# Four small reorderings where the attention of a fused attention, convolution-gate and channel-mix kernel hands over to its projections

## What is computed

```python
# 1. attention, 16 heads in all, masked by a hash bucket of q and k (6 bits)
mask = q_bucket[:, :, :, None] == k_bucket[:, :, None, :]
scores = np.where(mask, scale * np.matmul(q, k.transpose(0, 1, 3, 2)), -1e9)
attn = softmax(scores);  x = merge_heads(attn @ v)
# 2. gated projection: causal convolution over 5 tokens gives the gate
gate = sigmoid(sum_k conv_w[k] * x[t - 4 + k])
x = (gate * (x @ w_val)) @ w_out
# 3. channel mix with the previous token
xk = mu_k * x + (1 - mu_k) * x_prev;  xr = mu_r * x + (1 - mu_r) * x_prev
k = relu(xk @ w_k);  r = sigmoid(xr @ w_r)
out = r * ((k * k) @ w_v)
```

## Time and profile before

| | |
|---|---|
| runs of the kernel (3) | 488.40, 488.49, 489.15 us; median 488.49 |
| profiled execution | 488.57 us, its span 486.8 us |
| TensorE busy | 475.1 us, 98% of the span |
| VectorE, ScalarE, GpSimd busy | 350.5, 279.2, 257.9 us |
| granted TensorE clock | 1.00 in all stretches |

### The profile page before, as it was taken

How to read it: one execution, slowest core, us unless ns; L and a number is a source line. 1 busy time by engine, 2 the same in 40 slices (tenths; PEclk the granted TensorE clock), 3 DMA queues, 4 the chain that set the end, 5 groups by cost and what they waited for, 6 DMA issues and landing times.

```text
span 486.8 us, 9484 instructions
## 1 busy us (share of the span) xinstructions
PE 475.1 (98%) x3541; PEld 403.4 (83%) x3541; DVE 350.5 (72%) x611; ACT 279.2 (57%) x597; POOL 257.9 (53%) x254
## 2 busy tenths in 40 slices
PE   8899999999999999999999999999999999999997
PEld 6766677676676676667679998999999999999997
DVE  4887897988889888887687986884786588226211
ACT  4977878887787887876645533451442353244230
POOL 5795547284463746451267546464456458246140
PEclk9999999999999999999999999999999999999999
DMA  6210310304031030200220001001000000000101
GB/s 229 66 55 18 116 37 25 114 16 136 16 97 58 1 135 18 72 18 18 88 86 1 3 1 43 1 1 45 2 2 32 12 2 19 27 1 12 34 1 43
DMA packets 10557, 20.69 MB, mean 42 GB/s; under 512 B 1680, under 2 KB 6928, under 8 KB 10512
## 3 DMA queue, kind: packets, MB, share of 16 engines
q1 hardware_dynamic: 10224, 19.94, 12.5%
q10 hardware_dynamic: 288, 0.15, 0.1%
HBM read 16.94 MB, written 3.15 MB: 41 GB/s over the span
## 4 chain that ended last, share of the span: by engine, by line
PE 78%; DVE 11%; issue 4%; ACT 3%; DMA 2%; POOL 1%; SPq 0%; DVEq 0%; ACTq 0%; POOLq 0%
PE ps L717 28%; PE ps L705 14%; PE ps L725 12%; PE ps L681 10%; PE ps L670 10%; DVE gate L898 2%; DMA raw_k<-kT 2%; ACT probs L482 2%; PE ps L691 2%; DVE tmp_a L971 1%; DVE negmax L855 1%; DVE pt L862 1%; DVE tmp_b L969 1%; PE ps L653 1%; DVE x L888 1%
## 5 line engine op out<-in xcount | busy, mean ns | idle before, releaser
L855 DVE TENSOR_REDUCE negmax<-ps 128x1 f32<-128x768 f32 x96 | 91.7, 956 | 23.7 <-PE ps L670 22.6
L670 PE MATMUL ps<-k,q 128*128 128x384 f32 x384 | 91.9, 361 | 3.1 <-ACT probs L482 2.5
L482 ACT ACTIVATE probs<-ps,negmax 128x768 f32<-128x768 f32 x96 | 86.6, 902 | 9.8 <-DVE negmax L855 9.4
L681 PE MATMUL ps<-ident,probs 128*128 128x128 f32 x576 | 82.4, 275 | 1.9 <-ACT pt L490 0.7
L681 PEld LDWEIGHTS ps<-ident,probs 128*128 128x128 f32 x576 | 66.7, 140 | 12.8 <-DVE pt L862 4.7
L670 PEld LDWEIGHTS ps<-k,q 128*128 128x128 f32 x384 | 62.7, 189 | 14.8 <-ACT probs L482 10.2
L705 PE MATMUL ps<-pt,vals 128*64 128x384 f32 x384 | 68.8, 494 | 0.0
L436 POOL TENSOR_TENSOR h_lo<-tmp_b,h_hi 128x256 fp32r<-128x256 f32 x48 | 38.7, 812 | 45.9 <-ACT h_hi L584 45.9
L490 ACT ACTIVATE pt<-ps 128x384 f32<-128x384 f32 x96 | 47.0, 489 | 19.7 <-PE ps L681 15.9
L862 DVE COPY pt<-ps 128x384 f32<-128x384 f32 x96 | 52.2, 543 | 3.7 <-PE ps L681 3.7
L725 PE MATMUL ps<-h_hi,w_hi 128*128 128x256 f32 x192 | 54.3, 283 | 0.0
(11 more groups left out here) (87 smaller groups left out, 1124.8 us busy)
## 6 DMA issues: line engine op xcount, KB each, us to landing
w_raw<-w SPq DMA_DIRECT2D x8, 640.0 KB, 6.9
raw_q<-qT SPq DMA_DIRECT2D x8, 384.0 KB, 5.8
raw_k<-kT SPq DMA_DIRECT2D x8, 384.0 KB, 3.5
vals<-v SPq DMA_DIRECT2D x16, 192.0 KB, 2.3
out<-w_raw SPq DMA_DIRECT2D x24, 128.0 KB, 1.7
w_raw<-w SPq DMA_DIRECT2D x4, 512.0 KB, 3.2
codes_b<-codes ACTq DMA_DIRECT2D x1, 128.0 KB, 4.1
proj_bd<-proj ACTq DMA_DIRECT2D x1, 16.0 KB, 3.3
```

Of the source, the lines that this page charges most:

```text
L482: act.activation(probs[par][:, :], score[par], ACT.Exp, bias=negmax[:, t:t + 1], accum_out=sums[:, t, 0:1]).then_inc(exp_done, 1)
L670: last = pe.matmul(ps[:, 2 * par + half, 0:HALF], qq[h][:, q], kk[h][:, half * HALF:(half + 1) * HALF], start=first, stop=not first)
L681: last = pe.transpose(tbank[u][:, k * P:(k + 1) * P], probs[g % 2][:, kt * P:(kt + 1) * P], ident[:, :])
L855: dve.tensor_reduce(negmax[:, t:t + 1], score[g % 2], AX.XY, ALU.max, negate=True).then_inc(max_done, 1)
```

## The change

1. *Gate tile ahead of transposes (TensorE).* The first value tile of chunk 0 goes from behind the transposes of step 94 to behind those of step 93, so ahead of those of step 94. It gets a wait for the exponential of step 94, whose score banks it overwrites.
2. *Low parts on GpSimd.* The four low parts of y of chunk 0 go from VectorE to GpSimd, two ahead of each of its two pieces of w_v's low part.
3. *Keys do not wait for the receptance (TensorE).* `s_k` waits for seven of the eight low parts of the mixtures, `s_r` for all eight.
4. *Tanh behind the next second stage (ScalarE), left taps between outputs (VectorE).* `tanh_gate(c + 2)` goes behind `s_out(c + 1)`. The left taps (12 in chunk 0, 4 in chunks 1 to 3) go from the end of `s_k` into `s_v`: a quarter ahead of each output product.

```diff
@@ block.gpsimd
+            y_low(0, 0)
+            y_low(0, 1)
             w2_low(0)
+            y_low(0, 2)
+            y_low(0, 3)
             w2_low(1)
             pool.wait_ge(mm["val"], DT)
             x_low(1)
@@ block.scalar
+                if c + 1 < CHUNKS:
+                    s_out(c + 1)
                 if c + 2 < CHUNKS:
                     tanh_gate(c + 2)
-                if c + 1 < CHUNKS:
-                    s_out(c + 1)
@@ block.tensor
-                if i == LAST and t >= TILES - 2:
+                if i == LAST and t >= TILES - 3:
                     pe.wait_ge(xlo_done, 1)
-                    s_val_tile(0, 2 * (t % 2))
-                    s_val_tile(0, 2 * (t % 2) + 1)
+                    if t < TILES - 1:
+                        pe.wait_ge(exp_done, NHEADS * KT - 1)
+                        s_val_tile(0, t - (TILES - 3))
+                    else:
+                        s_val_tile(0, 2)
+                        s_val_tile(0, 3)
@@ s_k, s_r
-                pe.wait_ge(mixlo_done, (c + 1) * 2 * DT)
+                pe.wait_ge(mixlo_done, (c + 1) * 2 * DT - 1)
...
             def s_r(c):
+                pe.wait_ge(mixlo_done, (c + 1) * 2 * DT)
@@ block.vector
+            def tap_rate(c):
+                return 2 if c else 1
...
-                if c + 2 < CHUNKS:
-                    for n in range(taps * FT, DT * TAPS):
-                        convolve_tap(c + 2, n // TAPS, n % TAPS)
 
             def s_v(c):
-                dve.wait_ge(rec_done, c + 1)
+                left = DT * TAPS - tap_rate(c) * FT
                 for m in range(DT):
+                    if c + 2 < CHUNKS:
+                        for n in range(DT * TAPS - left + left * m // DT, DT * TAPS - left + left * (m + 1) // DT):
+                            convolve_tap(c + 2, n // TAPS, n % TAPS)
+                    if m == 0:
+                        dve.wait_ge(rec_done, c + 1)
                     dve.wait_ge(mm["v"], c * DT + m + 1)
...
             gated(0, 1)
             normalise(NHEADS - 2)
-            y_low(0)
-            y_low(1)
             gated(0, 2)
             gated(0, 3)
-            y_low(2)
-            y_low(3)
             normalise(NHEADS - 1)
```

More of the change, by code:

```diff
@@ L418, in gates, with y_low @@
                     .then_inc(gate_done, 1)
+            def y_low(c, m):
+                pool.wait_ge(yhi_done, c * DT + m + 1)
+                pool.tensor_tensor(y_lo[:, m, :], tmp_a[:, m % 2, :], y_hi[:, m, :], ALU.subtract)\
+                    .then_inc(ylo_done, 1)
             def s_val(c):
                 for m in range(DT):
-                    pool.wait_ge(yhi_done, c * DT + m + 1)
-                    pool.tensor_tensor(y_lo[:, m, :], tmp_a[:, m % 2, :], y_hi[:, m, :], ALU.subtract)\
-                        .then_inc(ylo_done, 1)
+                    y_low(c, m)
             def s_out(c):
@@ L955, in s_val @@
                     gated(c, m)
[L957 to L960, removed]
             def s_out(c):
@@ L982, in save_last @@
                     dve.memset(z[:, :, 0:1], 0.0).then_inc(hist_done, 1)
+            def tap_rate(c):
+                return 2 if c else 1
             def s_k(c):
-                taps = 2 if c else 1
+                taps = tap_rate(c)
                 for m in range(FT):
```

## The result

The changed kernel takes 485.91 us (median of 6 runs, 485.69 to 486.08) against 488.50 of the kernel before (6 runs): a ratio of 0.9944, 95% interval 0.9934 to 0.9954, 2.6 us or 0.5% faster.

The account below looks back on a forecast made before the run. TensorE was taken as the bound, with 2.5 us of waits to remove. Terms: -1.15 at the keys, -1.2 at chunk 2's value tiles, +0.6 new wait, sum -1.75 us, giving 486.8 us; range 486.0 to 487.9.

Parts of the forecast that it names:

- What bounds the kernel, and where the gains lie: TensorE bounds, busy 146.88 of 146.92 us from 337.25 us on; its three earlier waits, together 2.5 us, are the most to gain.
- Gate tile: TensorE, step 94's transposes: a value tile of 1.4 us fills the 0.67 us wait for a copy; gain 0.7 us.
- Low parts on GpSimd: Chunk 0's y low parts cost 0.74 us each on GpSimd, ready 1.6 us early; on VectorE all but 0.15 us is lost.
- The mixing chain moves 0.4 us, not 0.7: VectorE's first difference of chunk 0, held by GpSimd's x low part, ends at 252.9 instead of 253.26; keys start at 261.0.
- Tanh and taps, the gain: TensorE, first gate-value tile of chunk 2: output products come in time, so the 1.20 us wait goes; gain 1.2 us.
- New wait: 0.6 us: TensorE, output projection of chunk 2 near 317.6: waits for ScalarE's receptance tanh because the gate comes late; bounds 0 and 1.1.
- GpSimd in its own way: Rival, chance 0.07: y low parts on GpSimd take 1.21 us each, keys start 0.75 us later than before; 488.7 us.
- Taps held up: Rival, chance 0.05: the 12 taps between VectorE's outputs take 0.98 us each, new wait 6.2 us; 492.4 us.
- The gate eating the second gain: Rival, chance 0.14: the new wait at chunk 2's output projection is 1.1 us or more, start gives only 0.74; 487.7 us.

Follow-up runs that it names:

- the delayed gates: Changed kernel with two or five extra unused multiplications ahead of the last tap of chunk 0's output stage on VectorE: 486.50 us with two, 487.15 us with five.
- the two kernels with a wait near 2 us: The changed kernel without the tanh and taps moved (488.22 us), and the kernel before with only keys not waiting for the last receptance low part (490.37 us).

## Why the prediction was wrong

By its steps:

- **What bounds the kernel, and where the gains lie: right.** All three waits that it read the earlier trace rows are gone, the view of TensorE's waits has none beyond 340 us, and the gain changes there by less than 0.1 us (2.78 to 2.71).
- **Gate tile: right in kind, too small.** 0.87 us instead of 0.7. The term was the 0.67 us idle of the row, which counts from the modelled end of the transposes; a following matmul starts inside that end. From the start of step 93's transposes to what follows them it is 1.49 us before and 0.57 after, so the tile began 0.9 us ahead of where the next transposes had stood.
- **Low parts on GpSimd: the step failed.** The forecast had "Left on VectorE they would give the gap back but for 0.15 us". The run with them on VectorE gives L unchanged. I had taken the end of a chain (249.96) as a fixed time, though the instructions in it were held by GpSimd's weight pieces, and these followed the gates, the tanh and so TensorE: the whole chain moved 0.86 us. The forecast's time did not rest on this gap, since the low parts were moved; but the move put them ahead of the x low part in GpSimd's queue, and that is how the next step came to reckon 0.4 us.
- **"The mixing chain moves 0.4 us, not 0.7": failed by its size.** It moved 0.78 (27.61 to 26.83 into L). Of the 0.4 us more, 0.17 is the gates' earlier end (TensorE's larger gain), the rest GpSimd's durations: weight pieces at 2.4 instead of 2.45, neighbours overlapping. With it the keys gain 1.47 us instead of 1.15. Undoing the tile costs 0.89 us and undoing the keys' earlier start 0.74.
- **Tanh and taps, the gain: right in kind, too small.** 1.36 us for the 1.2, for the same reason as at the gate tile: the row's 1.20 counts from a modelled end. That the taps must move for it was not said there, and the runs show that they need not: the tanh alone gives 1.43 us in the kernel before, and with all else in place the taps are worth 0.36.
- **"New wait: 0.6 us": mis-sized.** It is 0.12. The mechanism is shown by the delayed gates, one for one. The term behind it, the gate's time, was 1.3 us late: 0.33 from two taps of 0.35 us counted at 0.51, 0.5 from durations summed where starts follow each other faster, and about 0.5 from the stage beginning earlier. TensorE could go on 83.46 us into L and not at the forecast's 84.4, and it was itself there 0.5 us earlier than reckoned.
- **The sum and the range.** The forecast of 1.75 us fell short of the 2.71 in L by 0.32 at the start, 0.16 at the second gap and 0.48 at the new wait: the new wait is half of the miss. The range's lower end stood on 1.35 at the start, 1.2 at the second gap and no new wait. The first was passed by 0.12 and the second, which had no bound of its own, by 0.16, and 0.12 came back at the wait.
- **The rivals.** GpSimd in its own way: ruled out by 0.72 us for a low part. Taps held up: ruled out, 0.5 each but for the first, which was held beside GpSimd's last low part as the forecast allowed (two took 1.56). The gate eating the second gain is the right mechanism, at a delay that the kernel does not have; 1.2 us more of it cost 1.2.

The sum in measured terms: -1.47 at the keys, -1.36 at the value tiles, +0.12 at the new wait and nothing left elsewhere: -2.71 in L, against 2.6 us between the medians.

What neither the forecast nor the waits of the kernel before told is how the parts hang together. The gate tile pays alone (0.75 us in L), because the mixing chain moves with it and so does everything on VectorE up to the output products. The tanh pays alone (1.43). The keys' part does not: the mixing chain and VectorE's taps behind it stay where they were, so the 0.70 us that TensorE won ahead of them came back as a longer wait behind, 1.8 to 2.1 us instead of 1.2, and in most executions the clock fell there. With the tile, the low parts and the keys together only the tile's 0.8 us arrives. Part 4 is what makes part 3 pay.

## What to carry to other kernels

Sum start-to-start steps, not durations, when a queue of short instructions sets a time: five of 0.35 us took 1.40, and twelve taps with three outputs came 0.5 us sooner than their durations say. Take each instruction's own row: the first tap of a tile was not like the others. Before a moment on another engine is taken as fixed, follow what released it; if that leads back to the engine that you speed up, it moves with it. Before an early wait is removed alone, ask whether the chain that ends the later wait moves with it. For the gate tile it did and all arrived; for the keys it did not, the later wait only grew, and behind the longer wait the lower clock cost more than the wait itself had grown.

## What was not expected of the hardware

TensorE's granted clock fell to 0.50, the lower of its two levels (1.2 GHz), behind single waits, with the engine busy before and behind: after waits of 1.79, 1.84 and 3.24 us. After one of 2.06 us and one of 1.20 us it stayed at 1.00. The price was 1.5 to 1.6 us each time: the four value tiles behind the wait took 7.22 to 7.26 us instead of 5.7. In the executions without a profile the mean granted clock tells the two kinds apart: five of twelve and eight of twelve had the lower one in the two kernels with a wait near 2 us, four of six in the one with 3.24 us. The kernel before, with its 1.20 us, is not free of it: of its 55 executions with a clock on record two, of 490.69 and 490.75 us, have a mean of 0.996, though no profile shows where in them. So the length of the wait alone does not decide it, and why one execution of a program has it and the next has not stays open. The Trainium skill, "TensorE: Matmul & The Clock Gate" (Part 1), has the clock follow how busy the engine has recently been. The profiled rows agree so far that the clock fell only behind a wait; which waits do it they do not tell. The changed kernel has no wait over 0.2 us in this part, and its six executions lie within 0.4 us.

A second observation is the held instruction. In the kernel with low parts on VectorE two subtractions of 0.38 us took 4.31 us beside GpSimd's weight pieces, and on GpSimd the same four ran undisturbed at 0.72. That cost nothing in either place here, since the queue behind them had the time. It did cost in the run with three extra multiplications: they took 2.20 us (0.89, 1.13 and 0.33 us, each overlapping the next) while GpSimd worked on a low part and the gate from 297.19 to 298.96, where five of the same took 1.40 us with GpSimd idle. These read one tensor from SBUF, not two, so the two-operand instructions are not the only ones to look at. That GpSimd held them fits the times, but no run separates it from another cause.
